# Pair 2's transfers, pair 1's values and tile 2's distances take other places in the start of an attention block

## The chip, the cores and the metric

The kernel runs on one core of a Trainium2 chip. The time is that of the whole kernel on the device, in microseconds (us), and smaller is better. Three runs of the kernel before are compared; its profile is one more execution.

## The reference, cut to what matters

Banded attention with a linear distance bias, then a token-mixing and channel block, then a gated channel block. All in float32.

```python
# q, k, v: 2 batches x 8 heads x 768 tokens x 64; n_global 8, n_local 96
scores = q @ k.T / 8 - slope[head] * dist     # masked outside the band of 96 and the 8 global keys
dist   = where(is_global & ~is_local, n_local, abs(rel))
x      = softmax(scores) @ v                  # heads laid side by side: 2 x 768 x 512
u      = x + ((x.T @ U) @ V).T                # rank 32, over the tokens
y      = u + relu(u @ w_ch1) @ w_ch2          # 512 -> 2048 -> 512
# then: x_prev = y shifted by one token; k = relu(mix(y) @ w_k)**2; out = sigmoid(mix(y) @ w_r) * (k @ w_v)
```

## The kernel before, in words

Two heads make a **pair**; there are 8 pairs (p = 0 to 7). A pair has 6 tiles of 128 tokens, and two tiles make a **unit**: 3 units in a pair, 24 in all (n = 0 to 23). A query tile sees a window of 192 keys, so each unit's scores are small matrix products, 64 x 192 at a time.

For each unit, in the order in which the engines pass it on: TensorE makes the scores (`scores`, L446); VectorE adds the distances and takes the row minimum of the negated scores (`maxima`, L909); ScalarE takes the exponentials (`exps`, L714); TensorE transposes the weights (`turn`, L460); VectorE and ScalarE copy one half each out of PSUM (`evac`, L918 and L722); TensorE multiplies them by the values (`weigh_rest`, L476, then `weigh`, L484); VectorE divides (`normalise`, L931). The stages of several units overlap: TensorE's written order at step n is `turn(n-2)`, `scores(n)`, `weigh_rest(n-3)`, `weigh(n-3)`. After the third unit of a pair TensorE also does the token mixing of that pair (`mixing`, L492, L507, L499). The order of the work on each engine is written out by hand; engines wait for one another on counting semaphores alone.

SyncE's queue issues nearly all transfers, in the written order, and a wait in it holds all that is queued behind. Per pair these are `load_qk` (queries 384 KB, L371, and keys 512 KB, L372, counted in `qk_in`), `load_rest` (384 KB of values, L375) and twice `load_main` (384 KB each, L378), counted in `v_landed`, and a few 256 KB pieces of the first weights (`load_piece`, L384). Queries, keys and values have two buffers each, picked by p % 2. `qk_done` counts the units whose scores are done. GpSimd scales the queries of pairs 1 to 7 (`prepare_pair`, L1112), and `scores` of a pair's first unit waits for that. `weigh_rest` of a pair's first unit waits for all three value transfers of the pair.

`dist` holds the four distance patterns of 192 columns that the tiles use. VectorE makes tile 0's and tile 1's at the start; GpSimd derives tile 2's and tile 3's from tile 1's (`more_distances`, L1096: one copy of 384 columns and eight small ones, counted in `dist_more`). `maxima(1)`, of unit 1, is tiles 2 and 3, and waits for these copies.

Behind the attention stand the channel products (L603, L615, L668, L683), long runs of 128 x 512 products on TensorE.

Of the kernel before, what the change touches and what calls it, by code (L numbers as in the profile page):

```python
# [17 lines left out]
P = 128  # L18
GLOB = 32
GROUP = 64  # L20
# [5 lines left out]
def block_kernel(nc, qt, kt_, vm, vr, k_plain, v_plain, counts, mix_u, mix_v, w_ch1, w_ch2, mus, w_k, w_v, w_r, out):  # L26
# [7 lines left out]


    PAIRS, _, S = qt.shape
    D = vm.shape[5]
    B, H = out.shape[0], out.shape[2] // D
# [21 lines left out]
    WIN = GLOB + SPAN  # L60
# [3 lines left out]
    def globs_at(g):  # L64
        return GROUP * (-g % 3)
# [13 lines left out]
    with ctx:  # L79
# [21 lines left out]
        def sem(name):  # L101
            return ctx.enter_context(nc.semaphore(name))
# [75 lines left out]
        dist = region("dist", [P, 4 * WIN])  # L178
# [38 lines left out]
        def score_bank(n, h):  # L217
            return bank[(FIRST_SCORE_BANKS[n] if n < UNITS else SCORE_BANKS)[h]]
# [13 lines left out]
        dist_more = sem("dist_more")  # L232
        counts_step = sem("counts_step")
        dist_step = sem("dist_step")
# [4 lines left out]
        qk_in = [sem(f"qk_in{i}") for i in range(2)]  # L239
        v_landed = [sem(f"v_landed{i}") for i in range(2)]  # L240
# [74 lines left out]
        def unit_tiles(n):  # L315
            return [(i, 2 * (n % UNITS) + i) for i in range(2)]
# [13 lines left out]
        def dist_of(i, t):  # L330
            at = WIN * (t % 3 or (3 if t else 0))
            return dist[:, at:at + WIN]

        def group(j):
            return slice(j * GROUP, (j + 1) * GROUP)
# [32 lines left out]
        @block.sync  # L368
        def _(sp):
            def load_qk(p):  # L370
                sp.dma_start(q_in[:, p % 2, :], qt[p]).then_inc(qk_in[p % 2], 16)  # L371
                sp.dma_start(k_in[:, p % 2, :], kt_[p]).then_inc(qk_in[p % 2], 16)  # L372

            def load_rest(p):
                sp.dma_start(v_rest[:, p % 2, :, :, :, :], vr[p]).then_inc(v_landed[p % 2], 16)  # L375

            def load_main(p, j):
                sp.dma_start(v_in[:, p % 2, j, :, :, :], vm[p][:, j, :, :, :]).then_inc(v_landed[p % 2], 16)  # L378

            def load_piece(k):  # L380
                c, t = divmod(k, 4)
                if k >= 2:
                    sp.wait_ge(piece_in[k % 2], 16 * (k // 2))
                sp.dma_start(raw[c][:, t * QF:(t + 1) * QF], chunks[c][0][:, t, :]).then_inc(piece_in[k % 2], 16)  # L384

            def load_chunk(c):
                sp.dma_start(raw[c % 2][:, :].rearrange("p (t n) -> p t n", t=4), chunks[c][0]).then_inc(raw_in[c % 2], 16)


            quarters = {2: (0,), 3: (1,), 4: (2, 3), 5: (4,), 6: (5,)}  # L390
            sp.dma_start(counts_i[:, :], counts.partition_broadcast(P)).then_inc(counts_in, 16)
            sp.wait_ge(qk_in[0], 32)
            load_rest(0)
            load_main(0, 0)
            load_main(0, 1)
            sp.wait_ge(qk_in[1], 32)
            sp.dma_start(U[:, :, :], mix_u).then_inc(uv_in, 16)
            sp.dma_start(V4[:, :], mix_v).then_inc(uv_in, 16)
            sp.dma_start(mu[:, :, :], mus).then_inc(mu_in, 16)
            sp.wait_ge(v_landed[0], 48)  # L400
            for p in range(1, PAIRS):
                sp.wait_ge(qk_done, UNITS * p)
                if p + 1 < PAIRS:
                    sp.wait_ge(qk_in[(p + 1) % 2], 32 * ((p + 1) // 2))
                    load_qk(p + 1)
                else:
                    load_piece(PIECES - 2)
                    load_piece(PIECES - 1)
                sp.wait_ge(qk_done, UNITS * p + 1)
                if p > 1:  # L410
                    sp.wait_ge(pv_done, UNITS * (p - 1))
                    sp.wait_ge(v_landed[p % 2], 48 * (p // 2))
                load_rest(p)
                load_main(p, 0)
                sp.wait_ge(qk_done, UNITS * p + 2)
                load_main(p, 1)
                for k in quarters.get(p, ()):
                    load_piece(k)
            for c in range(2, NCH):
                sp.wait_ge(split_w, c - 1)  # L420
                load_chunk(c)
            for t in range(NBLK * TPB):
                sp.wait_ge(result_done, TPB + t + 1)
                sp.dma_start(out_dram[:, t, :], result[:, t % TPB, :]).then_inc(stored[t % TPB], 16)
            for i in range(TPB):
                sp.wait_ge(stored[i], 16 * (NBLK + 1))
# [410 lines left out]
        def _(dve):  # L837
# [55 lines left out]
            for g in range(2 * GROUPS):  # L893
                q, at = group(g % 2), WIN * (g // 2) + globs_at(g)
                dve.tensor_tensor(dist[q, at:at + GLOB], dist[q, at:at + GLOB], glob_far[q, :],
                                  ALU.min).then_inc(dist_step, 1)

            def maxima(n):
                p = n // UNITS
                dve.wait_ge(qk_done, n + 1)  # L900
                if n == 0:
                    dve.wait_ge(dist_step, 6)
                for h in range(2):
                    if h == 1 and n >= 2:
                        dve.wait_ge(pt_done, 2 * (n - 2) + 2)
                    for i, t in unit_tiles(n):
                        if n == 1 and h == 0:
                            dve.wait_ge(dist_more, 5 + 4 * i)
                        m = dve.tensor_tensor_reduce(probs[:, n % 2, h, i * WIN:(i + 1) * WIN],  # L909
                                                     score_bank(n, h)[:, i * WIN:(i + 1) * WIN],  # L910
                                                     dist_of(i, t), slopes[2 * (p % PPB) + h], 3.0e38,
                                                     ALU.add, ALU.min, neg_max[:, n % 2, i, h:h + 1])
                    m.then_inc(max_done, 1)
# [22 lines left out]
            def banded_attention():  # L936
                for n in range(NU + 3):
                    if 2 <= n < NU + 2:
                        dve.wait_ge(pt_done, 2 * (n - 2) + 2)
                    if n >= 3:  # L940
                        denominators(n - 3)
                    if 2 <= n < NU + 2:
                        evac(n - 2)
                    if n < NU:
                        maxima(n)
                    if n >= 3:
                        normalise(n - 3)
# [103 lines left out]
            with dve.Fori(0, NBLK) as j:  # L1051
                for f in range(FT2):
                    g = FT2 * j + f
# [17 lines left out]
        def _(pool):  # L1071
# [21 lines left out]
            def more_distances():  # L1093

                def copy(to, frm):
                    pool.tensor_scalar(to, frm, 1.0, 1.0, ALU.mult, ALU.mult).then_inc(dist_more, 1)  # L1096

                pool.wait_ge(dist_step, 6)
                pool.wait_ge(q_scaled, 2)
                copy(dist[:, 2 * WIN:4 * WIN].rearrange("p (a c) -> p a c", c=WIN),  # L1100
                     dist[:, WIN:2 * WIN].unsqueeze(1).broadcast_to([P, 2, WIN]))
                pool.wait_ge(dist_more, 1)
                for g, to, frm, width in ((4, GROUP, GROUP + GLOB, GROUP), (4, P, GROUP, GLOB), (5, 0, GLOB, GROUP), (5, GROUP, 0, GLOB),
                                          (6, 0, GROUP, GLOB), (6, GLOB, 0, GROUP), (7, 0, GLOB, P), (7, P, 0, GLOB)):
                    q, at = group(g % 2), g // 2 * WIN + to
                    copy(dist[q, at:at + width], dist[q, WIN + frm:WIN + frm + width])
                pool.wait_ge(dist_more, 9)

            def prepare_pair(p):

# [45 lines left out]
            with pool.If(fast > 0):  # L1156
                more_distances()
                prepare_pair(1)
                for p in range(PAIRS):
                    if p + 2 < PAIRS:  # L1160
                        prepare_pair(p + 2)
                    for half in range(2):
                        if p >= 1:
                            split_u(p - 1, half)
                        if p == PAIRS - 2:
                            split_piece(p + half)
                    for k in {2: (0,), 3: (1,), 4: (2, 3), 5: (4, 5)}.get(p, ()):
                        split_piece(k)
# [110 lines left out]
```

## Time and profile before

| what | value |
|---|---|
| three runs | 521.35, 515.89, 516.37 us; median 516.37 |
| profiled execution | 514.89 us, span 513.0 us, so 1.9 us lie outside the span |
| TensorE busy | 501.4 us (98%) |
| VectorE, ScalarE, GpSimd busy | 182.4, 131.5, 241.9 us |
| granted TensorE clock | 0.999 |

The span runs from the first to the last instruction of the profiled execution. Times in rows are us from its start. PE is TensorE's products, PEld its weight loads, DVE VectorE, ACT ScalarE, POOL GpSimd, SPq SyncE's queue. In the chain of waits, "issue" is time in which the engine waited for nothing that the profile shows.

### The profile page before, as it was taken

To read this page: it belongs to the slowest core of one execution; us is meant where nothing else is said; L and a number is where in the kernel's file an instruction comes from. 1 tells how busy PE (TensorE), PEld (TensorE's weight loads), DVE (VectorE), ACT (ScalarE), POOL (GpSimd) and SP (SyncE) were. 2 spreads that over 40 slices of the span, in tenths; PEclk is the share of its full clock that TensorE was granted. 3 is DMA by queue.
4 is the path that set the end of the run, shared out by engine and by line. 5 is a ranking of instruction groups with operands and counts; after the bars stand their busy time and mean duration, and the time that the engine had idled before them with its cause. 6 is when DMAs were issued, how large, how long until landed. Compare 5 with 4: busy or idle time off the path is not lost.

```text
span 513.0 us, 9448 instructions
## 1 busy us (share of the span) xinstructions
PE 501.4 (98%) x3682; PEld 414.3 (81%) x3682; DVE 182.4 (36%) x477; ACT 131.5 (26%) x354; POOL 241.9 (47%) x234
## 2 busy tenths in 40 slices
PE   7799999999999999999999999999999999999997
PEld 5687787788888888888888888888888888888885
DVE  6787783131221313313133131320444243432223
ACT  5888793100101100011100101021312132212220
POOL 4146783191027000199400929971999489950000
PEclk9999999999999999999999999999999999999999
DMA  7888772022003100034400000000000200020002
GB/s 272 273 264 260 275 254 100 1 82 82 0 1 105 58 0 0 1 86 160 163 0 0 1 1 0 0 0 1 0 0 1 82 0 0 0 82 0 0 0 82
DMA packets 15343, 34.48 MB, mean 67 GB/s; under 512 B 1488, under 2 KB 1872, under 8 KB 15312
## 3 DMA queue, kind: packets, MB, share of 16 engines
q1 hardware_dynamic: 14448, 32.22, 18.7%
q10 hardware_dynamic: 864, 1.84, 1.0%
q8 instruction: 21, 0.34, 0.3%
q14 instruction: 10, 0.08, 0.0%
HBM read 30.91 MB, written 3.15 MB: 66 GB/s over the span
## 4 chain that ended last, share of the span: by engine, by line
PE 95%; issue 1%; DMA 1%; DVE 1%; ACT 1%; POOL 0%; ACTq 0%; POOLq 0%
PE psum L615 26%; PE psum L603 25%; PE psum L668 13%; PE psum L659 13%; PE psum L683 6%; PE psum L446 3%; PE psum L484 3%; PE psum L460 2%; PE psum L492 1%; PE psum L476 1%; PE psum L499 1%; DMA k_in<-in_k 1%; PE psum L507 1%; POOL dist L1096 0%; ACT probs L714 0%
## 5 line engine op out<-in xcount | busy, mean ns | idle before, releaser
L1017 DVE SCALAR_TENSOR_TENSOR HL<-psum,HH 128x512 fp32r<-128x512 f32 x48 | 33.2, 692 | 172.4 <-ACT HH L803 172.4
L803 ACT ACTIVATE HH<-psum 128x512 fp32r<-128x512 f32 x48 | 28.8, 599 | 229.5 <-PE psum L603 229.5
L615 PE MATMUL psum<-HH,w2h 128*128 128x512 f32 x192 | 75.1, 391 | 0.0
L603 PE MATMUL psum<-UH,w1h 128*128 (+1 forms) x192 | 74.8, 390 | 0.0
L615 PE MATMUL psum<-HH,w2l 128*128 128x512 f32 x192 | 74.7, 389 | 0.0
L615 PE MATMUL psum<-HL,w2h 128*128 128x512 f32 x192 | 74.7, 389 | 0.0
L603 PE MATMUL psum<-UL,w1h 128*128 (+1 forms) x192 | 74.7, 389 | 0.0
L603 PE MATMUL psum<-UH,w1l 128*128 (+1 forms) x192 | 74.7, 389 | 0.0
L1144 POOL TENSOR_SCALAR w1h<-raw 128x2048 fp32r<-128x2048 f32 x4 | 7.7, 1928 | 118.2 <-PE psum L615 118.2
L1055 DVE TENSOR_TENSOR k_square<-k_relu 128x512 f32<-128x512 f32 x24 | 23.9, 997 | 66.6 <-ACT k_relu L828 66.5
L714 ACT ACTIVATE probs<-probs,neg_max 128x192 f32<-128x192 f32 x96 | 42.5, 444 | 10.6 <-DVE neg_max L909 9.4
L615 PEld LDWEIGHTS psum<-HH,w2h 128*128 128x128 f32 x192 | 36.1, 188 | 8.0 <-issue 0.6
L615 PEld LDWEIGHTS psum<-HL,w2h 128*128 128x128 f32 x192 | 36.0, 188 | 7.6
L603 PEld LDWEIGHTS psum<-UL,w1h 128*128 128x128 f32 x192 | 36.0, 188 | 7.5
L603 PEld LDWEIGHTS psum<-UH,w1l 128*128 128x128 f32 x192 | 36.1, 188 | 7.5
L603 PEld LDWEIGHTS psum<-UH,w1h 128*128 128x128 f32 x192 | 36.0, 188 | 7.5
L615 PEld LDWEIGHTS psum<-HH,w2l 128*128 128x128 f32 x192 | 36.0, 188 | 7.3
L1026 DVE TENSOR_TENSOR Y<-psum,Y 128x512 f32 (+1 forms) x48 | 32.5, 692 | 26.5 <-PE psum L615 26.5
L668 PE MATMUL psum<-WVH,HH 128*128 128x512 f32 x96 | 37.3, 389 | 0.0
L668 PE MATMUL psum<-WVL,HH 128*128 128x512 f32 x96 | 37.3, 389 | 0.0
L668 PE MATMUL psum<-WVH,HL 128*128 128x512 f32 x96 | 37.3, 389 | 0.0
L1209 POOL TENSOR_SCALAR here<-Y,mu 128x512 f32<-128x512 f32 x24 | 20.4, 848 | 34.5 <-PE psum L683 22.4
(121 smaller groups left out, 859.2 us busy)
## 6 DMA issues: line engine op xcount, KB each, us to landing
v_in<-in_v SPq DMA_DIRECT2D x16, 384.0 KB, 4.7
raw<-in_moe_w_ch SPq DMA_DIRECT2D x6, 1024.0 KB, 5.0
v_rest<-in_v_rest SPq DMA_DIRECT2D x8, 384.0 KB, 3.9
k_in<-in_k SPq DMA_DIRECT2D x6, 512.0 KB, 5.5
out<-result SPq DMA_DIRECT2D x12, 256.0 KB, 2.1
q_in<-in_q SPq DMA_DIRECT2D x6, 384.0 KB, 3.9
raw<-in_moe_w_ch SPq DMA_DIRECT2D x8, 256.0 KB, 4.4
raw<-in_moe_w_v SPq DMA_DIRECT2D x2, 1024.0 KB, 5.2
```

The costliest lines, as they stand in the source:

```text
L446: mm = pe.matmul(score_bank(n, h)[group(j), i * WIN:(i + 1) * WIN], q_in[r, p % 2, t * P + j * GROUP:t * P + (j + 1) * GROUP], k_in[r, p % ...
L603: mm = pe.matmul(bank[4 + f % 2][:, 0:BLK], w[:, kt, f * P:(f + 1) * P], x[:, kt, ds(blk * BLK, BLK)], start=kt == 0 and n == 0, stop=kt = ...
L615: mm = pe.matmul(bank[d][:, 0:BLK], w[:, f, d * P:(d + 1) * P], x[:, f % 2, :], start=f == 0 and n == 0, stop=f == FQ - 1 and n == 2)
L659: mm = pe.matmul(bank[6 + f % 2][:, 0:BLK], w[:, kt, (f % 4) * P:(f % 4 + 1) * P], x[:, kt, ds(j * BLK, BLK)], start=kt == 0 and n == 0, s ...
L668: mm = pe.matmul(bank[t][:, :], x[:, f % 2, t * P:(t + 1) * P], w[:, f, :], start=f == 0 and n == 0, stop=f == FT2 - 1 and n == 2)
L683: mm = pe.matmul(bank[GATE_BANKS[t % 2]][:, :], x[:, kt, t * P:(t + 1) * P], w[:, kt, :], start=kt == 0 and n == 0, stop=kt == KT - 1 and ...
L714: e = act.activation(pr, pr, ACT.Exp, bias=neg_max[:, n % 2, i, h:h + 1], scale=-1.0, accum_out=sums[:, n % 4, i, h:h + 1])
L803: act.activation(HH[:, f % 2, :], bank[4 + f % 2][:, 0:BLK], ACT.Relu).then_inc(hid_high, 1)
L1017: dve.scalar_tensor_tensor(out=HL[:, f % 2, :], in0=bank[4 + f % 2][:, 0:BLK], scalar=0.0, in1=HH[:, f % 2, :].bitcast(F32), op0=ALU.max, ...
L1026: dve.tensor_tensor(y, bank[d][:, 0:BLK], y, ALU.add).then_inc(acc_added, 1)
L1055: dve.tensor_tensor(k_square[:, f % 2, :], k_relu[:, f % 2, :], k_relu[:, f % 2, :], ALU.mult).then_inc(square_done, 1)
L1209: pool.tensor_scalar(here[:, :], Y[:, d, at + 1:at + BLK + 1], mu[:, m, d:d + 1], 0.0, ALU.mult, ALU.add).then_inc(shift_step, 1)
```

## The change

Four things are edited. (1) SyncE no longer waits for pair 0's values before it issues pair 2's queries and keys. (2) Pair 1's values are issued only when pair 2's queries and keys landed. (3) From p = 2 on, the queries and keys of pair p + 1 are issued only when the values of pair p - 1 landed (at p = 7 it is the last two pieces of weights that wait). (4) Tile 2's four small copies go from GpSimd to VectorE, which does them between `maxima(0)` and `maxima(1)`; GpSimd keeps the wide copy and tile 3's four.

```diff
             sp.dma_start(mu[:, :, :], mus).then_inc(mu_in, 16)
-            sp.wait_ge(v_landed[0], 48)
             for p in range(1, PAIRS):
                 sp.wait_ge(qk_done, UNITS * p)
+                if p >= 2:
+                    sp.wait_ge(v_landed[(p - 1) % 2], 48 * ((p - 1) // 2 + 1))
                 if p + 1 < PAIRS:
                     sp.wait_ge(qk_in[(p + 1) % 2], 32 * ((p + 1) // 2))
                     load_qk(p + 1)
...
                 sp.wait_ge(qk_done, UNITS * p + 1)
+                if p == 1:
+                    sp.wait_ge(qk_in[0], 64)
...
+            def order_tile_2():
+                dve.wait_ge(dist_more, 1)
+                for g, to, frm, width in ((4, GROUP, GROUP + GLOB, GROUP), (4, P, GROUP, GLOB), (5, 0, GLOB, GROUP), (5, GROUP, 0, GLOB)):
+                    q = group(g % 2)
+                    dve.tensor_copy(dist[q, 2 * WIN + to:2 * WIN + to + width],
+                                    dist[q, WIN + frm:WIN + frm + width]).then_inc(dist_step, 1)
+                dve.wait_ge(dist_step, 10)
+
             def maxima(n):
                 p = n // UNITS
+                if n == 1:
+                    order_tile_2()
                 dve.wait_ge(qk_done, n + 1)
...
-                        if n == 1 and h == 0:
-                            dve.wait_ge(dist_more, 5 + 4 * i)
+                        if n == 1 and h == 0 and i == 1:
+                            dve.wait_ge(dist_more, 5)
...
-                for g, to, frm, width in ((4, GROUP, GROUP + GLOB, GROUP), (4, P, GROUP, GLOB), (5, 0, GLOB, GROUP), (5, GROUP, 0, GLOB),
-                                          (6, 0, GROUP, GLOB), (6, GLOB, 0, GROUP), (7, 0, GLOB, P), (7, P, 0, GLOB)):
+                for g, to, frm, width in ((6, 0, GROUP, GLOB), (6, GLOB, 0, GROUP), (7, 0, GLOB, P), (7, P, 0, GLOB)):
...
-                pool.wait_ge(dist_more, 9)
+                pool.wait_ge(dist_more, 5)
```

On SyncE's queue, from the last of the small tables (L399) to the queries of pair 4, the rows are these, `-` before and `+` now; `qk_in0` and `v_landed0` belong to the even pairs, `qk_in1` and `v_landed1` to the odd ones.

```order
 L399 DMA mu<-in_mu 128x8
-L371 DMA q_in<-in_q 128x768 [waits qk_in0,qk_done,v_landed0]
+L371 DMA q_in<-in_q 128x768 [waits qk_in0,qk_done]
 L372 DMA k_in<-in_k 128x1024
-L375 DMA v_rest<-in_v_rest 128x768 [waits qk_done]
+L375 DMA v_rest<-in_v_rest 128x768 [waits qk_in0,qk_done]
 L378 DMA v_in<-in_v 128x768
 L378 DMA v_in<-in_v 128x768 [waits qk_done]
-L371 DMA q_in<-in_q 128x768 [waits qk_in1,qk_done]
+L371 DMA q_in<-in_q 128x768 [waits qk_in1,v_landed1,qk_done]
 L372 DMA k_in<-in_k 128x1024
```

No transfer changes its place in the queue; what moved are the waits: off pair 2's queries, onto pair 1's values and onto pair 3's queries, and from there onto every later pair's queries in the same way.

On VectorE, between the last row of `maxima(0)` and the second tile of `maxima(1)`, the kernel before has

```order
L909 ISA neg_max 128x1
L909 ISA probs,neg_max<-psum,dist 128x192 [waits dist_more,qk_done]
L909 ISA neg_max 128x1
L909 ISA probs,neg_max<-psum,dist 128x192 [waits dist_more]
L909 ISA neg_max 128x1
```

and the changed kernel

```order
L924 ISA neg_max 128x1
L907 COPY dist<-dist 64x64 [waits dist_more]
L907 COPY dist<-dist 64x32
L907 COPY dist<-dist 64x64
L907 COPY dist<-dist 64x32
L924 ISA probs,neg_max<-psum,dist 128x192 [waits qk_done,dist_step]
L924 ISA neg_max 128x1
L924 ISA probs,neg_max<-psum,dist 128x192 [waits dist_more]
L924 ISA neg_max 128x1
```

so four copies stand on VectorE ahead of the first tile of unit 1, and that tile waits for them in place of GpSimd's first five. (L909 is L924 in the changed file.) TensorE's and ScalarE's rows are the same in both.

## Rows read from the trace of the kernel before

**Rows 1.** The page: the chain that ended last, by engine.
```profile
PE 95%; issue 1%; DMA 1%; DVE 1%; ACT 1%; POOL 0%; ACTq 0%; POOLq 0%
```

**Rows 2.** Window of the attention's middle: stretch, its us, busy us (instructions) of PE, PEld, DVE, ACT, POOL, clock, DMA share, GB/s.
```profile
21.20:40.00 18.80, 18.68 (x490) 16.04 (x493) 15.37 (x76) 15.02 (x59) 7.55 (x11) 1.00 0.81 249
```

**Rows 3.** The chain of waits, first 100 us: start, length, what.
```profile
19.11 2.11 issue
...
50.78 0.42 issue
...
61.55 0.98 issue
...
82.28 5.67 PE psum L603 x24
```

**Rows 4.** DMA queues (packets, MB, share) in 13.4:18.7, 18.7:19.9, 60.1:61.2.
```profile
q1 hardware_dynamic: 601, 1.74, 93.3%
...
q8 instruction: 1, 0.02, 5.4%
...
q8 instruction: 1, 0.02, 5.3%
```

**Rows 5.** Windows between the stalls, 21.23 to 51.22 and 51.22 to 62.54.
```profile
21.23:51.22 29.99, 29.30 (x754) 24.67 (x754) 23.83 (x120) 24.54 (x97) 14.90 (x19) 1.00 0.83 254
51.22:62.54 11.32, 10.28 (x253) 8.54 (x253) 8.64 (x40) 9.44 (x36) 7.73 (x10) 1.00 0.89 311
```

**Rows 6.** Windows of 1 us around pair 2's transfers.
```profile
12.70:13.70 1.00, 1.00 (x38) 0.86 (x34) 0.73 (x3) 1.00 (x7) 0.00 (x0) 1.00 0.40 97
13.70:14.70 1.00, 0.23 (x8) 0.12 (x6) 1.00 (x8) 1.00 (x5) 0.00 (x0) 1.00 0.71 144
14.70:15.70 1.00, 1.00 (x27) 0.91 (x31) 0.93 (x6) 1.00 (x6) 0.00 (x0) 1.00 1.03 383
```

**Rows 7.** Timeline of SyncE's queue, 9 to 57 us: start, length, issue.
```profile
9.26 0.88 SPq L399 DMA_DIRECT2D mu<-in_mu  x1
12.69 0.33 SPq L371 DMA_DIRECT2D q_in<-in_q  x1
29.20 0.33 SPq L371 DMA_DIRECT2D q_in<-in_q  x1
...
56.29 0.33 SPq L371 DMA_DIRECT2D q_in<-in_q  x1
```

**Rows 8.** DMA issues, us to landing: L378's at 16.09, 26.46, 53.55, 63.47; L372's at 29.57.
```profile
v_in<-in_v SPq DMA_DIRECT2D x1, 384.0 KB, 5.6
v_in<-in_v SPq DMA_DIRECT2D x1, 384.0 KB, 4.4
v_in<-in_v SPq DMA_DIRECT2D x1, 384.0 KB, 3.9
v_in<-in_v SPq DMA_DIRECT2D x1, 384.0 KB, 3.2
k_in<-in_k SPq DMA_DIRECT2D x1, 512.0 KB, 6.6
```

**Rows 9.** Timeline of all engines, to 40 us; in brackets idle time, and its releaser.
```profile
3.91 0.17 DVE L862 COPY reach<-reach 64x32 f32<-64x32 f32 x1
7.15 2.57 POOL L1096 TENSOR_SCALAR dist<-dist 128x384 f32<-128x384 f32 x9 [1.81 <-ACT q_in L760]
8.82 0.36 DVE L909 CUSTOM_DVE_ANT_0 probs<-psum,dist 128x192 f32<-128x192 f32 x1 [0.41 <-POOL dist L1096]
9.76 0.36 DVE L909 CUSTOM_DVE_ANT_0 probs<-psum,dist 128x192 f32<-128x192 f32 x1 [0.57 <-POOL dist L1096]
10.16 0.46 ACT L714 ACTIVATE probs<-probs,neg_max 128x192 f32<-128x192 f32 x1 [0.41 <-DVE neg_max L909]
22.48 0.43 PEld L476 LDWEIGHTS psum<-v_rest,probs_t 64*64 64x64 f32 x16
39.66 0.46 PEld L476 LDWEIGHTS psum<-v_rest,probs_t 64*64 64x64 f32 x16
```

## The prediction

> **What bounds the kernel now.** I read the chain of waits by engine first: 95% of it is TensorE [rows 1]. The window of the attention's middle says the same, 18.68 of 18.80 us [rows 2]. The channel products follow the attention with no gap, from 82.28 on [rows 3]. Nothing in the change touches them, so what it can gain or lose is the time at which TensorE comes to 82.28, and every us there is a us of the end.
>
> The holes are in the chain itself: three stretches called issue, in which TensorE waited for nothing that the profile shows, 2.11 us at 19.11, 0.42 at 50.78, 0.98 at 61.55 [rows 3]. The first falls inside a run of `weigh` products, where no semaphore is waited for. The DMA queues tell more: in the 5.3 us before it queue q1 moves 601 packets of data and queue q8, of kind instruction, none; the one packet of q8 comes in 18.7 to 19.9, and TensorE goes on at 21.22. Another stands in 60.1 to 61.2, ahead of the end of the third hole at 62.53 [rows 3, 4]. And the holes stand at even distances in TensorE's own count: 754 + 754 products and weight loads from the end of the first to the end of the second, 253 + 253 to the end of the third, 2.98 to 1; times are 29.99 and 11.32 us, 2.65 to 1 [rows 5]. I read this as TensorE running out of instructions: blocks of a fixed size come by DMA, each is asked for as the one before is begun, and when the DMA engines are full of data it comes late. At 13.4, just where q8 is silent for 5.3 us, the queue had been given pair 2's queries at 12.69 and keys, and pair 1's values behind them, to 16.09 [rows 7, 8].
>
> A rule of the Trainium skill speaks against this (Runtime: NRT & Kernel Launch, Instruction fetch mechanics): instructions come in blocks of 16 KiB or 256, TensorE holds 2048 of them, and the fetch is said to be mostly hidden. The block size agrees, since 1508 and 506 records are 5.9 and 2.0 blocks; a store of 2048 doesn't, since three holes would not be there. By the rule the holes are something else, and the time is that of the fourth rival below, 516.0 in place of 514.7.
>
> **Pair 2's transfers.** Their issue is held to 12.69 by pair 0's values; SyncE is free from 9.26 + 0.88 = 10.14 [rows 7], and the scores of unit 2, the wait that is left, are long done. So they are issued 2.55 us sooner. The DMA engines have room for them: 97 and 144 GB/s in the two us from 12.70 on, against 383 at 14.70 [rows 6], which is 239 + 286 = 0.53 MB of room. What was issued ahead drains to about 12.7; then 384 + 512 KB, 0.92 MB, take 2.4 us at 383 GB/s, to 15.1. The keys' issue, at 10.52, plus the 4.4 to 5.6 us in which most in [rows 8] landed gives 14.9 to 16.1; I take 15.7. Pair 2 is needed first by the scores of unit 6, half a us ahead of `weigh_rest(3)` (22.48 before [rows 9], 19.97 at the soonest, below), and GpSimd needs 0.9 to scale it, so there are 2.9 us of slack and by itself this gains nothing.
>
> **Pair 1's values behind them.** They go out at about 15.8, 16.2 and 16.6, in place of 13.5, 14.0 and 16.09: the last one, which counts, 0.5 us later. What this buys is a short queue in front of TensorE's block that is asked for at about 13.4: 0.9 MB in place of the 1.74 that passed before q8's packet [rows 4]. With the packet behind 15.1 to 16.1 and the same 21.22 - 19.9 = 1.3 us from its end to TensorE, the block is there at 17.5 to 18.5, and TensorE needs it at 19.11 - 0.4 = 18.7. The hole of 2.11 us goes; bounds for what goes of it are 0 (the hole is not the queue's) and 2.11. What is late next are the values: TensorE comes to `weigh_rest(3)` at 22.48 - 2.11 - 0.4 = 19.97 (the 0.4 is worked out below) and the last transfer must have landed. An issue of L378 took 3.2, 4.4 or 5.6 us to land [rows 8], so 19.8, 21.0 or 22.2. I take 4.4, since at 16.6 only two others of the same pair are ahead, while 5.6 had pair 2's and pair 3's around it and 3.2 was nearly alone. `weigh_rest(3)` then starts at 21.1 in place of 22.48 [rows 9]: **gain 1.4 us, between 0.2 and 2.5**.
>
> **Tile 2 by VectorE.** GpSimd's nine copies take 2.57 us, and VectorE stood 0.57 us for them before the second tile of `maxima(1)`; ScalarE then stood 0.41 for VectorE [rows 9]. Now VectorE does four copies of 0.17 us or less [rows 9] and one wait for them, some 0.65 us from 8.82 - 0.41 = 8.41 on, in which it stood idle before [rows 9]; `maxima(1)` begins at 9.05 in place of 8.82, but has no wait inside, since GpSimd has five copies left (7.15 + 2.57 less four small ones of a ninth of that each, 8.6). Its second tile comes at 9.35 and not 9.76, and ScalarE starts at 10.16 - 0.41 = 9.75, where it had ended `exps(0)`. ScalarE is busy from there to the copy that `turn(2)` waits for, so 0.4 us reach TensorE. That is the 0.4 above; it is inside the 1.4 and not added, since the values decide there. Bounds: 0 to 0.4, and below nothing down to -0.2, the later begin.
>
> **Later queries wait for values.** For pair 4 the issue at 29.20 [rows 7] moves to the landing of pair 2's values, 26.46 + 4.4 = 30.9 [rows 8]: 1.7 later, and for pair 7 the one at 56.29 to 53.55 + 3.9 = 57.5, 1.2 later; the others lie alike. Queries have slack: pair 4's keys landed at 29.57 + 6.6 = 36.2 [rows 8], GpSimd scales in 0.9, and the scores of unit 12 begin half a us ahead of `weigh_rest(9)` at 39.66 [rows 9]. So 1.7 is covered by 2.0, thinly. Behind the new wait SyncE has the next values, and whoever waits for those is `weigh_rest`. Two effects, of opposite sign:
> - The bytes bunch. Queries, keys and values now go out one behind the other, and the last value transfer of pair 2 had little room: it landed at 30.9, and `weigh_rest(6)` stands halfway between 22.48 and 39.66 [rows 9], at 31.1. If 0.92 MB of queries and keys stand 1.7 us later before it, it can be up to 1.5 late there and as much at pair 3, if that is alike, and TensorE's next block too. Bounds 0 to 3; I take 0.7, nearer nothing, because DMA engines that move 249 GB/s there [rows 2] reach 383 when full [rows 6].
> - The hole at 61.55. It ends the second of two blocks that take 11.32 us from 51.22 on [rows 5], so its block was asked for near the middle, 56.9, with pair 7's queries issued at 56.29 [rows 7] and the keys behind them. They now go at 57.5, after it. The 0.98 us [rows 3] should go; bounds 0 to 1.4, with the 0.42 before it.
>
> Net: 1.4 + 1.0 - 0.7 = **1.7 us**. Own time of the profiled execution 514.89, so 513.2 against it. It lies 1.5 under the median of the three runs, 516.37, and I forecast a median: **514.7**.
>
> **Rivals.**
> - *The values take the hole's place.* Pair 1's last transfer takes 5.6 us, lands at 22.2, and TensorE waits for it from 19.97 on: 0.2 us gained, with the later effects even, 516.2. For it: the transfers really are 0.5 us later. Against: less is queued around them.
> - *Bunching decides.* Pairs 2 to 4 find their values late, 1.5 us each at pairs 2 and 3 and 0.1 at the next, 3.1 in all, against a gain of 1.4 at the start and none at 61.55: +1.7, or 518.1, slower than before. It turns slower from the point at which value waits and new holes after 25 us sum to over 1.4 us (2.4, if the 0.98 goes). For it: 30.9 against 31.1. Against: TensorE's blocks meet shorter queues while the queries are held back.
> - *More holes close.* The start gains 2.5 and both later holes go: 516.37 - 2.5 - 1.4 = 512.5. For it: the same mechanism in all three. Against: the start needs a landing in 3.2 us.
> - *The hole isn't the queue's.* The 2.11 us stay wherever they come from, and only ScalarE's 0.4 us reach the end: 516.0. For it: no row names the cause of "issue". Against: the counts in [rows 5] and q8's packet just before each end. By a rule of the skill (DMA: Bandwidth & Descriptors, Queues, rings and completion order: an engine takes turns between its queues, packet by packet) the block would not stand behind q1's data, and shorter queues would not help it; 601 packets of q1 before one of q8 speak against that here.
>
> **How the numbers follow.** Forecast 45% (513.6 to 515.7), values in the hole's place 18%, more holes close 14%, bunching 13%, hole not the queue's 10%. The range to hold 8 in 10 takes in 512.5 of the third and 516.2 of the first, and part of bunching; single runs of one kernel lie some us apart (515.89 and 516.37, and one at 521.35), so 512.2 to 517.8. One per cent, 5.2 us, is about what a measurement of this kernel can tell from no change. A gain of 5.2 would need more than 2.5 + 1.4 us of known holes: 2%. A loss of 5.2 needs bunching at every pair: 4%. Within: 94%.
>
> **What the profile after would show.** Right: queries of pair 2 issued near 10.2, values of pair 1 near 15.8 to 16.6; a packet of q8 before 16.5 and no issue stretch of over 0.3 us near 19; TensorE waiting for the landing of the values before `weigh_rest(3)`, near 21; the second tile of `maxima(1)` near 9.35 and no wait for GpSimd; the issue stretch near 60 gone; L603 of the channel products first at about 80.6. Wrong if the hole of 2 us stands at the same count of products, if L603 comes first later than 82.3, or if TensorE waits for values at units 6, 9 and 12.

## The result: 0.56% slower, and the profile after

| | before | changed |
|---|---|---|
| median | 516.37 us (19 runs, 513.34 to 521.35) | 519.04 us (19 runs, 515.74 to 524.17) |
| ratio | 1 | 1.0056, 95% interval 1.0035 to 1.0078 |
| profiled execution | 514.89 us, span 513.0 | 518.18 us, span 516.1 |

Ratios are of runs within 1.5% of the fastest of the same kernel, which leaves out one run of the changed kernel here (524.17) and, further down, two of e2's twelve (520.86, 522.14), two of e10's and one of e5's. So 2.9 us were lost, 1.8 to 4.0, where 1.7 were to be gained. The time lies above the stated range, which ended at 517.8.

The changed kernel's page and its chain of waits, against [rows 1] and [rows 3] (L924 was L909, L480 was L476, L496 was L492, L607 was L603):

```profile
PE 96%; DMA 2%; issue 1%; DVE 0%; ACTq 0%; SPq 0%
...
7.33 7.02 DMA v_in<-in_v
...
16.98 1.49 PE psum L450 x16
...
32.35 0.26 issue
...
37.15 0.93 issue
...
48.71 0.77 issue
...
64.04 0.49 issue
...
79.22 0.89 issue
...
85.38 5.67 PE psum L607 x24
```

TensorE is still nearly the whole chain. The channel products start at 85.38, not 82.28: 3.1 us, which is the growth of the span, 516.1 less 513.0. All of it is lost in the attention. The hole of 2.11 us at 19.11 is gone, as forecast, and so is nearly all of the one that was 0.98 (here 0.49 at 64.04). But there are four others, and the run of products of one unit's scores takes 1.49 us at 16.98, where the same run takes 0.81 at 20.31.

SyncE's queue, against [rows 7]:

```profile
9.00 2.01 SPq L398 DMA_DIRECT2D V<-in_moe_V  x1
...
11.61 0.36 SPq L371 DMA_DIRECT2D q_in<-in_q  x1
12.01 0.43 SPq L372 DMA_DIRECT2D k_in<-in_k  x1
18.07 0.33 SPq L375 DMA_DIRECT2D v_rest<-in_v_rest  x1
...
23.35 0.33 SPq L371 DMA_DIRECT2D q_in<-in_q  x1
...
32.57 0.33 SPq L371 DMA_DIRECT2D q_in<-in_q  x1
```

Pair 2's queries went out at 11.61, not 10.2: an issue ahead of them took 2.01 us of SyncE's time. Pair 1's values went at 18.07, not 15.8: the keys were issued at 12.01, not 10.52, and took 6.0 us to land, not 5.2. Landings of three of L378 and L372, in the order 12.01 (keys), 18.93 and 27.21 (last values of pairs 1 and 2), against [rows 8]:

```profile
k_in<-in_k SPq DMA_DIRECT2D x1, 512.0 KB, 6.0
...
v_in<-in_v SPq DMA_DIRECT2D x1, 384.0 KB, 4.4
...
v_in<-in_v SPq DMA_DIRECT2D x1, 384.0 KB, 5.3
```

So pair 1's values landed at 18.93 + 4.4 = 23.3, and pair 2's at 27.21 + 5.3 = 32.5. The timelines of VectorE, TensorE's products and its weight loads show what waited, against [rows 9]:

```profile
8.27 0.62 DVE L907 COPY dist<-dist 64x64 f32<-64x64 f32 x4
8.93 0.36 DVE L924 CUSTOM_DVE_ANT_0 probs<-psum,dist 128x192 f32<-128x192 f32 x1
9.21 0.35 DVE L924 CUSTOM_DVE_ANT_0 probs<-psum,dist 128x192 f32<-128x192 f32 x1
...
14.39 0.71 PE L480 MATMUL psum<-v_rest,probs_t 64*64 64x64 f32 x16 [2.09 <-DMA v_in<-in_v]
...
23.36 0.35 PEld L480 LDWEIGHTS psum<-v_rest,probs_t 64*64 64x64 f32 x16 [0.24 <-issue]
...
32.58 0.35 PEld L480 LDWEIGHTS psum<-v_rest,probs_t 64*64 64x64 f32 x16 [0.58 <-issue]
```

The first number in brackets is the idle time ahead. VectorE's four copies took 0.62 us and the second tile of `maxima(1)` came at 9.21, not 9.76, with no wait: tile 2's part went as forecast. TensorE then stood 2.09 us for pair 0's values. `weigh_rest(3)` and `weigh_rest(6)`, at 23.36 and 32.58, start 0.06 behind the landings just read, so both waited for their values, though the trace calls those waits issue. The waits are short: from the unit before to `weigh_rest(3)` is 2.58 us (20.78 to 23.36), where it is 2.31 in e6 below, and to `weigh_rest(6)` 3.03 (29.55 to 32.58), where it is 2.27 in the kernel before. In the kernel before they started at 22.48, 0.8 behind a landing at 16.09 + 5.6, and near 31.1, 0.2 behind one at 30.9.

Last, two windows of the changed kernel: from 14.40 to 19.80, and the stretch from `weigh_rest(3)` to the first channel product.

```profile
14.40:19.80 5.40, 5.40 (x94) 4.57 (x96) 2.55 (x14) 2.45 (x11) 0.91 (x1) 0.53 0.46 157
...
23.36:85.30 61.94, 58.12 (x1484) 48.31 (x1480) 45.42 (x224) 48.72 (x187) 38.26 (x48) 1.00 0.77 258
```

The same stretch in the kernel before:

```profile
22.48:82.20 59.72, 57.46 (x1491) 48.28 (x1480) 45.52 (x224) 47.77 (x185) 38.19 (x48) 1.00 0.77 248
```

61.94 against 59.72 us for the same products: 2.2 of the 3.1 us are lost there, where edit 3 acts, and 0.9 before it. In the first window the clock is at 0.53 of full; profiles of the kernel before, further down, show that this is not the change's.

### The profile page after: what moved, and what is told of

Read it like the earlier page. It is cut to its first block, busy times and chain, and to the rows that moved or that the text cites. A ratio compares the mean times of both kernels' runs of the same rounds, so it can differ in the third digit from the quotient of the medians.

```text
span 516.1 us, 9449 instructions
## 1 busy us (share of the span) xinstructions
PE 503.7 (98%) x3682; PEld 415.6 (81%) x3682; DVE 183.4 (36%) x481; ACT 131.7 (26%) x354; POOL 241.6 (47%) x230
## 4 chain that ended last, share of the span: by engine, by line
PE 96%; DMA 2%; issue 1%; DVE 0%; ACTq 0%; SPq 0%
PE psum L619 25%; PE psum L607 25%; PE psum L672 13%; PE psum L663 13%; PE psum L687 6%; PE psum L450 3%; PE psum L488 3%; PE psum L464 2%; PE psum L480 1%; DMA v_in<-in_v 1%; PE psum L496 1%; PE psum L503 1%; DMA k_in<-in_k 1%; PE psum L511 1%; DVE probs L924 0%
## 5 line engine op out<-in xcount | busy, mean ns | idle before, releaser
L607 PE MATMUL psum<-UH,w1h 128*128 (+1 forms) x192 | 74.8, 390 | 0.0
L607 PE MATMUL psum<-UL,w1h 128*128 (+1 forms) x192 | 74.7, 389 | 0.0
L607 PE MATMUL psum<-UH,w1l 128*128 (+1 forms) x192 | 74.7, 389 | 0.0
L607 PEld LDWEIGHTS psum<-UL,w1h 128*128 128x128 f32 x192 | 36.1, 188 | 7.5
L607 PEld LDWEIGHTS psum<-UH,w1h 128*128 128x128 f32 x192 | 36.0, 188 | 7.6
L607 PEld LDWEIGHTS psum<-UH,w1l 128*128 128x128 f32 x192 | 36.0, 188 | 7.4
```

The lines of the kernel that those rows point to most:

```text
L607: mm = pe.matmul(bank[4 + f % 2][:, 0:BLK], w[:, kt, f * P:(f + 1) * P], x[:, kt, ds(blk * BLK, BLK)], start=kt == 0 and n == 0, stop=kt = ...
```

## The experiments

Each is set against runs of the kernel before on the same chip; "us" are the ratio's distance from 1 times its median there, near 516. The theories: **the hold costs** (edit 3, later queries wait for values), against **the start costs** (edits 1 and 2).

### Each part alone

```diff
 # e1: edit 3 alone
                 sp.wait_ge(qk_done, UNITS * p)
+                if p >= 2:
+                    sp.wait_ge(v_landed[(p - 1) % 2], 48 * ((p - 1) // 2 + 1))
 # e2: edits 1 and 2 alone
-            sp.wait_ge(v_landed[0], 48)
...
+                if p == 1:
+                    sp.wait_ge(qk_in[0], 64)
 # e3: order_tile_2 alone (edit 4)
 # e4: the changed kernel without e1's lines (edits 1, 2 and 4)
```

> The kernel before with the later queries held alone (edit 3: from p = 2 on, pair p + 1's queries wait for pair p - 1's values). If holding them is what costs (the bytes bunch, TensorE's blocks of instructions and the values come later), this is slower by some 2 to 3 us, near the whole 2.9 of the changed kernel. If the start is what costs, it is within 0.7 us of the kernel before. By the prediction it would be 0.3 us faster (1.0 less 0.7).

> The kernel before with the start's transfers alone (edits 1 and 2: pair 2's transfers without the wait for pair 0's values, pair 1's values behind them). If the start is what costs (pair 0's last values land late, TensorE stands, and its clock falls to half for some us), this is slower by 2 to 3 us. If only the held queries cost, it is faster by about 1.4 us, as predicted.

> The kernel before with tile 2's four copies on VectorE alone (edit 4). The second tile of the second unit starts 0.4 us sooner. Expected gain 0 to 0.4 us; if pair 0's values decide when TensorE goes on at 12.8, then it makes TensorE stand 0.4 us longer before them and gives 0.4 back behind them.

> The changed kernel without the held queries (edits 1, 2 and 4). If holding them costs, this is 2 to 3 us faster than the changed kernel, so about as the kernel before or 1.4 us faster. If the start costs, it is as slow as the changed kernel, 2 to 3 us over the kernel before.

| kernel | median, us | ratio (95%) | us |
|---|---|---|---|
| e1 hold | 518.41 | 1.0061 (1.0032 to 1.0089) | +3.1 |
| e2 start | 514.84 | 0.9989 (0.9955 to 1.0022) | -0.6 |
| e3 tile 2 | 515.07 | 0.9991 (0.9965 to 1.0017) | -0.5 |
| e4 start and tile 2 | 517.23 | 1.0034 (1.0003 to 1.0066) | +1.8 |

The hold alone is as slow as the whole change. e2 speaks against the start theory: it is not slower. e2 and e3 are each within the noise of no effect. e4 is slower than their sum, 0.9980, and its interval begins just above 1, so some loss by edits 1, 2 and 4 together isn't ruled out; I have no cause for it.

e2's profile shows the order that edits 1 and 2 make, as in the changed kernel. Its queue had the keys at 11.62 and pair 1's values only at 17.84:

```profile
11.62 0.44 SPq L372 DMA_DIRECT2D k_in<-in_k  x1
...
17.84 0.33 SPq L375 DMA_DIRECT2D v_rest<-in_v_rest  x1
```

In all three profiles with edits 1 and 2 (changed, e2, e4) the chain has no issue stretch of over 0.1 us between 15 and 21; but `weigh_rest(3)` starts at 23.36, 23.16 and 21.99, against 22.48, 22.19, 22.75 and 22.45 in four profiles of the kernel before (below). So the hole near 19 is not in them, and TensorE still comes to `weigh_rest(3)` no sooner in two of the three. Whether the edits took the hole away is another matter: it is missing without them too, and the clock tells where (under "What repeats from profile to profile"). The forecast had q8's packet before 16.5; it started at 17.56, 16.51 and 16.24.

### Small transfers

```diff
 # e6: for pairs 2 to 7
-  q_in[:, p % 2, :] ... k_in[:, p % 2, :] ... v_rest[:, p % 2, :, ...] ... v_in[:, p % 2, j, :, ...]
+  a quarter of the columns of q_in and k_in, one of 3 units of v_rest, two of 6 tiles of v_in
 # e7: the same with e1's lines;  e5: the kernel before, unchanged
```

> The kernel before once more, unchanged. Its profile tells which parts of the first one repeat. If the hole of 2.11 us at 19.11 is a feature of the kernel, it stands at the same count of TensorE's instructions here; if it hangs on how the DMA engines happened to run, it is elsewhere or smaller, and the holes at the other even distances change too. The time is that of the kernel before, within 0.5 us.

> The kernel before with small transfers: of pairs 2 to 7 only a quarter of the queries and keys and a third of the values are loaded, with the same issues, waits and semaphores; the rest of the buffers keeps old data. If the holes called issue come from the load on the DMA engines, none is left from pair 2 on and the time falls by 2 to 3 us. If they are a matter of TensorE's own, they stay and the time is that of the kernel before.

> The kernel with small transfers and the later queries held (edit 3). If what edit 3 costs comes from bytes that stand one behind the other (late values, late blocks of instructions), it costs nothing here, within 0.5 us of the one with small transfers alone. If it costs by the wait itself (SyncE comes later to what is behind it), it is 1 to 3 us slower than that one.

e5: 516.45 us, ratio 0.9979 (0.9946 to 1.0012). This is what an unchanged kernel can show: the interval is 1.7 us wide to either side, and smaller effects aren't told apart here. e6: 511.36 us, 0.9898 (0.9861 to 0.9936), 5.3 us faster. e7: 511.74 us, 0.9910 (0.9875 to 0.9944). The means of these 6 and 7 runs are 0.2 us apart (511.37 and 511.58). So the hold costs next to nothing when the transfers are small, and 3.1 us when they are whole: it costs by bytes, not by the wait.

Below is the whole stretch from `weigh_rest(3)` to the first channel product in e6, as a window:

```profile
23.07:80.03 56.96, 56.42 (x1492) 47.91 (x1484) 45.36 (x224) 48.58 (x189) 38.41 (x48) 1.00 0.42 123
```

The DMA share is 0.42 in place of 0.77, and 56.96 us is what this stretch takes when nothing is late. Its chain has no issue stretch over 0.1 us but the 0.26 at the end of the attention, which every kernel has; e7's is the same. So all holes of this stretch are the DMA engines' doing, and the kernel before loses 59.72 - 56.96 = 2.8 us there, the changed one 5.0.

### The other order

```diff
 # e8: the hold, and for p = 2 to 6 the queries of pair p + 1 behind the first two values of pair p
+                    sp.wait_ge(v_landed[(p - 1) % 2], ...)
                 load_rest(p)
                 load_main(p, 0)
+                if 1 < p < PAIRS - 1:
+                    load_qk(p + 1)
```

> The kernel before with the later queries held, and issued behind the next pair's first two value transfers in place of ahead of them (pairs 2 to 6). If edit 3 costs since values stand behind queries and keys, this takes back most of its 3.1 us: within 1 us of the kernel before. If it costs since TensorE's blocks of instructions come later when much is issued at once, the bunch is as large as before and this stays 2 to 3 us slower.

522.13 us, 1.0120 (1.0079 to 1.0162): 6.2 us slower, worse than the hold. Queries became the new wait; a row of the waits of TensorE and one of GpSimd:

```profile
PE psum L451 <- POOL q_in L1117: 4.1, 5, 1.2
...
POOL q_in L1117 <- DMA k_in<-in_k: 37.5, 6, 10.3
```

TensorE waited 4.1 us for scaled queries. It tells that queries may not go much later, and so nothing on how the hold's 3.1 us split.

### Where the hold costs

```diff
 # e9:  if p == 2:   e10: if p >= 3:   in place of e1's p >= 2
 # e11: the third value transfer right behind the second
-                sp.wait_ge(qk_done, UNITS * p + 2)
                 load_main(p, 1)
 # e12: e11 and e1's lines
```

> The kernel before with the hold at p = 2 alone: only pair 3's queries wait, for pair 1's values. There the move is the largest (about 3.6 us, 18.3 to 21.9) and pair 2's values, which had 0.3 us of room, are behind. If late values of pair 2 are the cost, this is 1 to 2 us slower than the kernel before; if the cost is spread over all pairs, about a sixth of 3.1, 0.5 us.

> The kernel before with the hold at p = 3 to 7 alone. If late values of pair 2 are the cost, this is within 1 us of the kernel before; if it is spread over all pairs, it is 2 to 3 us slower.

> The kernel before, but the third value transfer of each pair is issued right behind the second, without its wait for the scores of the pair's second unit (some 3 us sooner). If values that land too late set TensorE's time, this is 0.5 to 2 us faster. If a bunch of transfers is what costs, by late blocks of instructions, it is 1 to 3 us slower.

> The hold at all pairs (edit 3) with that sooner third value transfer. If the hold costs since values land late, most of its 3.1 us comes back: within 1 us of the kernel before. If it costs by the bunch in front of TensorE's blocks of instructions, it stays 2 to 4 us slower.

| kernel | median, us | ratio (95%) | us |
|---|---|---|---|
| e9 hold at pair 3 | 517.02 | 1.0023 (0.9993 to 1.0054) | +1.2 |
| e10 hold from pair 4 on | 516.21 | 1.0003 (0.9968 to 1.0038) | +0.2 |
| e11 values sooner | 516.77 | 1.0022 (0.9994 to 1.0050) | +1.1 |
| e12 hold, values sooner | 519.31 | 1.0061 (1.0030 to 1.0092) | +3.1 |

e9 and e10 are inside the noise; their sum, 1.4 us, is below e1's 3.1, but the intervals allow 3.1. More of it seems to be at pair 3's queries, which isn't shown. e11, values sooner without the hold, gains nothing. e12, the hold with values sooner, is 3.1 us over the kernel before, as e1 is, and 2.0 over e11, a difference that the two intervals leave open. In its profile `weigh_rest(6)` starts at 32.11, 0.6 behind its values. So late values of pair 2 aren't needed for the loss.

### What repeats from profile to profile

> The kernel before, unchanged, for one more profile. Measured against the small-transfer kernel's 57.0 us from the first values of pair 1 in use (weigh_rest(3)) to the first channel product, the kernel before lost 2.7 and 5.0 us so far. If the two that the hold adds are real, it stays between 2 and 5; and TensorE does not wait for pair 2's values.

> The hold alone (edit 3) once more, for its profile. If late values of pair 2 are a part of the cost, TensorE starts weigh_rest(6) within 0.1 us of their landing here too, 0.6 us or more later than the 8.6 us of a free pair. If only the blocks of instructions cost, it starts well after the landing, and the holes sum to 2 us more than in the kernel before.

> As e13: the kernel before, unchanged, a loss of 2 to 5 us in that stretch, and no wait for pair 2's values.

> As e14: the hold alone, a loss of 5 to 7 us in that stretch; with late values as a part, weigh_rest(6) within 0.1 us of the landing.

From each profile: start of `weigh_rest(3)` and of the first channel product (timeline of the weight loads), and what the stretch between takes over e6's 56.96 us.

| profile | `weigh_rest(3)` | channel products | loss, us |
|---|---|---|---|
| before | 22.48 | 82.20 | 2.8 |
| e5 before | 22.19 | 84.16 | 5.0 |
| e13 before | 22.75 | 83.17 | 3.5 |
| e15 before | 22.45 | 82.21 | 2.8 |
| changed | 23.36 | 85.30 | 5.0 |
| e1 hold | 21.99 | 84.73 | 5.8 |
| e14 hold | 22.39 | 84.26 | 4.9 |
| e16 hold | 22.73 | 87.55 | 7.9 |

Means 3.5 and 5.9: 2.4 us more with the hold, near its 3.1. Two of the eight hold a second thing: in e5 and e14 the clock was at 0.50 for some us of the stretch, from 28.0 and from 21.4.

The hole that the prediction built on does not repeat. Chains of waits of the four profiles of the kernel before, holes over 0.3 us between 15 and 72: first before, 2.11 at 19.11, 0.42 at 50.78, 0.98 at 61.55 [rows 3]. Then e5 and e15, from 22 on (ahead of it they have 0.47 at 19.28 and 1.67 at 19.26):

```profile
26.03 1.81 issue
...
63.33 1.34 issue
```

```profile
26.28 0.99 issue
...
61.09 1.65 issue
```

and e13:

```profile
36.07 1.14 issue
...
56.85 0.40 issue
...
62.29 0.44 issue
```

Only the one near 62 is in all four.

The hole near 19 goes by the clock. The pages have a line of the granted clock in 40 slices of some 13 us, in tenths. Of the kernel before, the first profile and e15 have the upper line here, with the hole (2.11 and 1.67); e13 has the lower one, without it, and so has e1, in which the hold has not acted yet at 19:

```profile
PEclk9999999999999999999999999999999999999999
...
PEclk9799999999999999999999999999999999999999
```

The same 5.3 us as a window, before and e1:

```profile
13.70:19.00 5.30, 4.53 (x125) 3.91 (x121) 5.16 (x28) 5.18 (x22) 0.91 (x1) 1.00 0.97 351
...
13.70:19.00 5.30, 5.30 (x88) 4.53 (x88) 4.34 (x22) 4.28 (x18) 0.91 (x1) 0.53 0.95 329
```

The DMA engines are as full in both, and q8's packet starts at 18.78 and 18.29. In e1, at half clock, TensorE comes to the end of its block at 20.67 and finds the next one there, 2.4 us behind the start of the packet; before, it came at 19.11 and had to stand until 21.22, also 2.4 behind it. All 20 profiles agree: in seven the clock was full from 11 to 20 us, and six of these have the hole (before, e5, e15, e11, e14, e16; not e12); in thirteen it was at half for some us there, and none has it, among them the changed kernel, e2 and e4, and e3, e6, e9, e10, e13 and e17 without edits 1 and 2. So no profile tells whether edits 1 and 2 close the hole at full clock.

With the hold, e1 and e16 from 30 on:

```profile
31.14 0.54 issue
...
36.66 0.93 issue
...
48.21 0.76 issue
...
58.66 0.99 issue
```

```profile
31.98 0.82 issue
...
48.52 1.04 issue
...
73.68 0.66 issue
...
79.65 0.88 issue
...
85.68 1.60 issue
```

The one near 62 is gone in both, and in e14; in the changed kernel 0.49 is left of it. In its place all four profiles with the hold at all pairs have one near 48 (0.77, 0.76, 0.77 in e14, 1.04), where the kernel before has 0.12 or none, and more at other places. It costs more than the issue stretch: from `weigh_rest(9)` to `weigh_rest(12)` these four take 10.02 to 10.30 us, the kernel before 9.24 and three times 8.60. It isn't the hold's alone, though: e4, without the hold, has 0.67 at 46.84, and e12, with it, has none there and costs as much.

Late values play a small part. `weigh_rest(6)` starts 0.06 us behind the landing of pair 2's values in the changed kernel, e1 (32.08) and e14 (32.06), but TensorE's way there from the unit before took 3.03, 3.56 and 2.32 us where 2.27 is free: up to 0.8 us in the changed kernel, as much in e1 beside its hole of 0.54, nothing in e14 and e16. `weigh_rest(9)` starts 0.5 us or more behind its values in all four.

What the hold does to the blocks can be counted. From the first instruction of one of TensorE's blocks of 256 (see the last section) to the start of q8's next packet, the mean of the twelve blocks from 26 us on, in us:

| kernel | profiles | mean, each profile |
|---|---|---|
| before | before, e5, e13, e15 | 2.11, 1.98, 1.76, 1.92 |
| with the hold | changed, e1, e14, e16 | 2.47, 2.66, 2.36, 2.76 |
| small transfers, without and with the hold | e6; e7 | 0.92; 1.10 |

With the hold a block comes some 0.6 us later on the mean, with no overlap between the two groups, and with small transfers a whole us sooner. e12 has 2.41. e4 has 2.91 without the hold, in a run of 520.03 us where its median is 517.23: single executions can differ by as much.

### A version for the hole near 62

```diff
 # e17: if p == 6:  in place of e1's p >= 2;   e18: the same with order_tile_2
```

> The kernel before with the hold at p = 6 alone: pair 7's queries wait for pair 5's values. In four profiles of the kernel before there was a hole at the same place of TensorE's instructions near 62 (0.98, 1.34, 0.44, 1.65 us); with the hold at all pairs it was 0, 0, 0 and 0.49. If a block of instructions comes late by what is issued just ahead of it, that hole goes here too and the time is 0.5 to 1.3 us lower. If the holes only follow the total load, it is unchanged.

> The same with tile 2's copies on VectorE as well. If both are real and add, 0.7 to 1.6 us lower than the kernel before; if tile 2's part is nothing, as e17.

e17: 516.00 us, 1.0017 (0.9975 to 1.0058). e18: 516.62 us, 1.0011 (0.9977 to 1.0045). No gain. In e17's profile the hole near 62 is gone and a larger one stands earlier, at the block before it; in e18's it is there as ever. Their chains:

```profile
57.73 1.43 issue
```

```profile
46.90 1.04 issue
...
62.56 0.98 issue
```

TensorE also waited for pair 7's values in e17, which landed at 79.43, 0.06 ahead of `weigh_rest(21)`:

```profile
77.97 1.55 issue
```

The kernel before has such a wait in e13 too (0.99 at 76.57), so this need not be the hold's. In these two profiles, pushing one pair's queries past one block moved the hole or left it. No version found beats the kernel before.

## Why the prediction was wrong

- **Where TensorE's time decides: right.** From the channel products to the end of the span it is 430.8 us before and now; all that was lost was lost ahead of them.
- **The holes are late blocks of instructions: right**, and more firmly than it was argued. With small transfers there is none (e6), and in 20 profiles the holes of the attention that no wait explains stand at whole multiples of 256 of TensorE's instructions (last section).
- **Pair 2's transfers and pair 1's values: not shown, and no gain seen.** The hole of 2.11 us is in none of the three profiles with these edits, but all three had half clock there, and with half clock it is in no profile of any kernel. It was also one draw: in other profiles of the kernel before it is 0.47 (e5), 1.67 (e15) or nothing (e13). Of the terms, the drain of what was issued ahead, put at 12.7, went on to the landing of pair 0's values at 14.34 (12.67 to 13.71 in the four profiles of the kernel before, but 14.24 in e10, where these edits aren't either), the keys landed at 18.0, not 15.7, and so pair 1's last values at 23.3, not 21.0. The transfer itself took the 4.4 us that were forecast; the first rival had the late landing, but by 5.6 us in transfer. Against a forecast gain of 1.4, e2 gained 0.6, from 2.3 gained to 1.1 lost, which leaves the 1.4 possible, and e4, with tile 2, lost 1.8, at least 0.2. I took a gain from a stretch of one execution.
- **Tile 2: right in the trace, nothing in the time.** 9.21 and not 9.76, no wait for GpSimd; e3 shows 0.5 us or nothing. TensorE then waited 2.09 us for pair 0's values, a wait that the prediction did not have.
- **Later queries wait for values: this is the step that failed.** It summed to a gain of 0.3 us (1.0 for the hole at 61.55 less 0.7 for bunching) and is a loss of 3.1 (e1; 1.6 to 4.6). The 1.0 was there: that hole is 0 to 0.5 in four profiles. The 0.7 was mis-sized; it must be near 4. The bound, 3, counted late values of two pairs. What the runs show in its place is that mostly other blocks of instructions come late: 0.6 us each on the mean, with holes near 37 and 48 in all four profiles and at two to five further places, and with late values of pair 2 beside them in two of four, 0.8 us at most. The prediction named this ("and TensorE's next block too") and priced it at nothing. The reason given for being near nothing, that the DMA engines have room at 249 GB/s on average, is a mean: a block is late by what is in front of it at one moment. That the hold makes those moments fuller is the reading that fits e6 and e7; no run shows it moment by moment.
- **The rival of bunching** had 13% and 518.1 us; the measured 519.04 is nearest to it, 0.9 beyond. Its way there, values late by 1.5 us at pairs 2 and 3, is not what the profiles show: 0.8 at most at pair 2, and none at pair 3. That its number came near is luck in part.

How the 3.1 us split between late blocks and late values stays open in numbers: the losses of single profiles spread by 3 us, and half clock behind a long hole is in some of them.

## What to carry to other kernels

A hole in one profile is one draw: where holes come from the load on shared DMA engines, take two or three profiles of the same kernel before pricing one, and price the load, not the hole. When transfers take most of the DMA engines' time (0.77 of it here), a wait that holds one transfer back does not thin the load but bunches it, and whatever else needs the same engines, TensorE's instructions too, comes late at another place. A copy of the kernel with small transfers, same waits, tells in one run what all of this can be worth: 5.3 us here. And compare the granted clock before calling a hole closed: here the one near 19 is in no profile in which TensorE ran at half clock ahead of it.

## What the runs showed of the hardware

TensorE's instructions come in blocks, and late ones stop it at even distances in its own count. In the changed kernel the windows between the ends of the holes near 37, 48 and 64 hold

```profile
38.09:49.48 11.39, 10.57 (x252) 8.52 (x253) 8.46 (x40) 9.30 (x37) 7.73 (x10) 1.00 0.78 268
49.48:64.54 15.06, 14.53 (x378) 12.39 (x379) 11.96 (x60) 12.54 (x51) 10.28 (x13) 1.00 0.82 267
```

505 and 757 products and weight loads, 2 to 3; before it was 506 and 1508 [rows 5], 1 to 3, all of them whole numbers of some 252. With TensorE's semaphore instructions counted too, as the traces keep them, it is exact: from the end of the hole at 19.11 to that at 50.78 and to that at 61.55 the kernel before has 1536 and then 512, and in all 20 profiles each hole of over 0.15 us from 15 us on that no semaphore and no landing ends stands at a multiple of 256. TensorE goes on 2.2 to 3.5 us after the start of a packet of queue q8, of kind instruction, and 1.1 to 1.6 after its end. The Trainium skill (Runtime: NRT & Kernel Launch, Instruction fetch mechanics) has blocks of 256 instructions, with which this agrees. The Trainium skill's statement there that the fetch is hidden since the engine dispatches more slowly than the store fills does not hold here while the DMA engines are loaded: 5.4 us of holes in one attention from 26 us on (e16).

The granted clock fell to half, 1.2 GHz, for some us near the start in 13 of the 20 profiles. In the changed kernel TensorE stood from 12.30 to 14.39, and the windows of 1 us read 0.98, then 0.50:

```profile
11.70:12.70 1.00, 0.40 (x6) 0.26 (x6) 0.48 (x4) 1.00 (x7) 0.00 (x0) 0.98 0.81 247
12.70:13.70 1.00, 0.00 (x0) 0.00 (x0) 0.96 (x5) 1.00 (x6) 0.00 (x0) 0.50 0.94 310
```

One unit's scores then took 1.49 us, and 0.81 after 20. The profile of the kernel before had a mean clock of 0.999, but its other runs range from 0.990 to 1.000, and e13 has the same fall at 12.9, so this is not the change's. It fell later too, behind long holes: in e5 after 1.81 us at 26.03, in e14 after 1.56 at 19.10, in e4 after 1.43 at 79.05, but not after the 2.11 at 19.11. A profile has half clock or the hole near 19, never both, and the runs at 1.000 are not the fastest of them (513.40 to 517.41 us, beside 512.36 at 0.993).
